# Attention and mixer kernel on one core: the second pair's q is half rotated on VectorE, and the third pair's q is loaded later on SP's queue

## The reference

```python
def rotate(x):
    x1, x2 = (x[..., :half], x[..., half:])
    return np.concatenate([x1 * cos - x2 * sin, x1 * sin + x2 * cos], axis=-1)
q_rot, k_rot = (rotate(q), rotate(k))
scores = scale * np.matmul(q_rot, k_rot.transpose(0, 1, 3, 2))
scores = scores - np.max(scores, axis=-1, keepdims=True)
attn = np.exp(scores)
attn = attn / (np.sum(attn, axis=-1, keepdims=True) + 1e-09)
return np.matmul(attn, v).astype(np.float32)
# mixer
xt = x.transpose(0, 2, 1)
h = np.maximum(xt @ w_tok1, 0.0) @ w_tok2
u = x + h.transpose(0, 2, 1)
h2 = np.maximum(u @ w_ch1, 0.0) @ w_ch2
return (u + h2).astype(np.float32)
```

## Time and profile before

| | us |
|---|---|
| median of three runs | 641.61 |
| the three runs | 641.15, 641.61, 1245.69 |
| profiled execution | 640.87 |
| its span, first to last instruction | 639.1 |
| PE busy / share of the span | 621.5 / 97% |
| DVE busy | 509.4 / 80% |
| ACT busy | 464.2 / 73% |
| POOL busy | 341.0 / 53% |

### The profile page before, as it was taken

How to read it: one execution, slowest core, us unless ns; L and a number is a source line. 1 busy time by engine, 2 the same in 40 slices (tenths; PEclk the granted TensorE clock), 3 DMA queues, 4 the chain that set the end, 5 groups by cost and what they waited for, 6 DMA issues and landing times.

```text
span 639.1 us, 13808 instructions
## 1 busy us (share of the span) xinstructions
PE 621.5 (97%) x4724; PEld 604.7 (95%) x4724; DVE 509.4 (80%) x877; ACT 464.2 (73%) x1016; POOL 341.0 (53%) x316
## 2 busy tenths in 40 slices
PE   3899999999999999999999999999999999999997
PEld 3799999999999999999999999999999999999997
DVE  6899999999999999987385985569935499553895
ACT  3889999988889899986383664776556765567753
POOL 3999999998888887560900002860017800068200
PEclk9999999999999999999999999999999999999999
DMA  4767766767668774406001332000320002100002
GB/s 133 168 159 197 212 151 179 187 173 183 174 176 211 203 189 114 122 20 216 19 1 44 155 84 75 1 2 2 84 74 0 0 0 80 43 33 1 1 3 74
DMA packets 61898, 63.01 MB, mean 99 GB/s; under 512 B 18896, under 2 KB 46160, under 8 KB 61840
## 3 DMA queue, kind: packets, MB, share of 16 engines
q1 hardware_dynamic: 61392, 62.15, 35.7%
q10 hardware_dynamic: 448, 0.10, 0.1%
HBM read 31.46 MB, written 9.44 MB: 64 GB/s over the span
## 4 chain that ended last, share of the span: by engine, by line
PE 95%; SPq 1%; DVE 1%; DMA 1%; ACT 0%; issue 0%; ACTq 0%; DVEq 0%
PE slot L615 12%; PE rest L648 12%; PE rest L625 9%; PE slot L1344 8%; PE slot L1346 8%; PE slot L1345 8%; PE rest L1344 6%; PE rest L1346 6%; PE rest L1345 6%; PE rest L376 3%; PE rest L576 3%; PE rest L635 2%; PE slot L1376 2%; PE rest L1376 2%; PE rest L224 1%; PE rest L221 1%
## 5 line engine op out<-in xcount | busy, mean ns | idle before, releaser
L1335 POOL TENSOR_TENSOR w_ch_part<-w_ch_sums,w_ch_part 128x512 fp32r<-128x512 f32 x21 | 31.0, 1474 | 173.3 <-ACT w_ch_part L1588 173.3
L984 DVE TENSOR_REDUCE neg_max<-slot 128x1 f32<-128x576 f32 x142 | 106.7, 752 | 6.6 <-PE slot L615 2.2
L1652 ACT ACTIVATE pieces<-h 128x288 fp32r<-128x288 f32 x168 | 73.8, 444 | 49.8 <-PE slot L1346 25.3
L992 DVE TENSOR_TENSOR pt_lo<-rest,pt_hi 128x512 fp32r<-128x512 f32 x144 | 96.0, 677 | 1.9 <-ACT pt_hi L845 1.3
L648 PE MATMUL rest<-pt_hi,v 128*128 128x256 f32 (+1 forms) x320 | 89.3, 303 | 0.0
L845 ACT ACTIVATE pt_hi<-rest 128x512 fp32r<-128x512 f32 x144 | 84.1, 595 | 5.2 <-PE rest L625 4.3
L1743 DVE TENSOR_TENSOR pieces<-h,pieces 128x288 fp32r<-128x288 f32 x168 | 74.6, 454 | 9.4 <-ACT pieces L1652 8.9
L648 PE MATMUL rest<-pt_lo,v 128*128 128x256 f32 (+1 forms) x256 | 69.7, 295 | 0.0
L615 PE MATMUL slot<-key,q_hi 128*128 128x288 f32 x252 | 63.5, 333 | 2.2 <-ACT prob_a L838 1.0
L838 ACT ACTIVATE prob_a<-slot,neg_max 128x576 f32<-128x576 f32 x78 | 58.0, 743 | 10.1 <-DVE neg_max L984 10.0
L648 PEld LDWEIGHTS rest<-pt_hi,v 128*128 128x128 f32 x320 | 60.3, 188 | 0.1
(11 more groups left out here) (263 smaller groups left out, 2107.3 us busy)
## 6 DMA issues: line engine op xcount, KB each, us to landing
key<-t_hi_k SPq DMA_DIRECT2D x31, 144.0 KB, 2.3
key<-t_lo_k SPq DMA_DIRECT2D x31, 144.0 KB, 2.4
raw_qk<-in_q_dram SPq DMA_DIRECT2D x16, 256.0 KB, 2.8
raw_v<-in_v_dram SPq DMA_DIRECT2D x16, 256.0 KB, 3.3
x_scratch<-x_pair SPq DMA_DIRECT2D x16, 256.0 KB, 2.1
stage_or_x<-x_scratch SPq DMA_DIRECT2D x16, 256.0 KB, 4.3
q_hi<-t_hi_q SPq DMA_DIRECT2D x31, 128.0 KB, 2.4
q_cross<-t_hi_q SPq DMA_DIRECT2D x31, 128.0 KB, 2.4
```

The costliest lines, as they stand in the source:

```text
L984: dve.tensor_reduce(neg_max[p % 2][:, i:i + 1], slot[g if 2 <= g < 4 else g % 2][:, :, 0:HALF], AX.XY, ALU.max, negate=True).then_inc(maxe ...
L992: dve.tensor_tensor(pt_lo[:, :, cols], rest[:, bank, :].rearrange("p (j n) -> p j n", j=G), f32(pt_hi[:, 0:G, cols]), ALU.subtract).then_i ...
L1652: act.activation(pieces[:, ring(m), 0, :], source[WEIGHTS[n]][:, ft, :], ACT.Copy).then_inc(piece_hi, 1)
```

## The change

`rotate` is cut in two: the products stay in `rotate`, the difference and sum become `rotate_halves`, which `rotate` calls itself except for the second pair's q (m = LENT = 3). There DVE calls it, behind the sixth maximum of the first pair, and POOL waits for `rotated` instead, before it goes on to v. On SP, `load_next("q", 2)` moves from before the loop to behind the second pair's set 0 tiles.

```diff
+    LENT = 3
@@
         eng.tensor_tensor(by_sin[:], x[:], sin, ALU.mult).then_inc(products, 1)
+        if m != LENT:
+            rotate_halves(eng, n, p)
+
+    def rotate_halves(eng, n, p):
+
+        m, half = 2 * p + "kq".index(n), D // 2
         eng.wait_ge(products, m * 2 + 2)
         if p > 0:
             eng.wait_ge(t_ready[n], p)
@@
         load_next("k", 2)
-        load_next("q", 2)
@@
             assemble_q(0, p + 1)
+            if p == 0:
+                load_next("q", 2)
             load_next("k", p + 3)
@@
         rotate(pool, "k", 1)
         rotate(pool, "q", 1)
+        pool.wait_ge(rotated, 2 * LENT + 2)
@@
-        for i in range(1, 7):
+        for i in range(1, 6):
             maximum(0, i)
+        rotate_halves(dve, "q", 1)
+        maximum(0, 6)
         t_part_lo("k", 1, 0)
```

## The result

The change made the kernel slower by 0.8 us: 641.91 us median of 20 runs, against 641.13 of 20 for the kernel before, ratio 1.0013 with a 95% interval of 1.0007 to 1.0019. That is 0.1%, far inside the 2% that the chances speak of, but neither interval includes 1. One of before's 20 runs, at 1245.69 us, is of another kind and enters no ratio. The profiled execution of after took 642.29 us, 640.2 of it span; of before, 640.87 and 639.1.

The account below looks back on a forecast made before the run. The prediction took PE as the chain from 28 us on, its earlier stall coming from SP's issuing. A gain of 0.45 less 0.05 is 0.4 us, from the 641.2 mean to 640.8, range 640.0 to 641.9.

Parts of the forecast that it names:

- the chances: Whole kernel, against a 2% (12.8 us) threshold: 0.01 faster, 0.98 same, 0.01 slower.
- the chain and the head: PE bounds from 28 us on; SP's earlier second-pair tiles shorten PE's early stalls, gaining 0.45 us at the third tile.
- the maximum: DVE's seventh maximum: pushed by the two added instructions from 19.73 to about 20.02, 0.29 us later.
- the high part of q: ACT's instruction for the second pair's q: starts at 21.54 instead of 21.66, only 0.12 us earlier.
- 0.45 less 0.05 is 0.4 us: The forecast's sum: gain at PE's 28.83 wait less the thin-cover allowance, with 0 to 0.6 us as bounds.
- The 0.05 for tiles that land late: Second half of the second pair's tiles: 0.05 us taken off because their cover is only 0.2 us.
- as long as no new wait arises: PE from 28 us on: time won before that point moves the end by the same amount, on this condition.
- The next wait of SP, ahead of the second pair's v and for POOL's split of the first, absorbs the shift on SP.: SP's queue after the second pair's second half: its later issues are made up at this wait.
- the cover of the second pair's second half: Last tile issued at 31.20, landing 33.6 at the median; PE wants it at 33.8, so 0.2 us, the thinnest.
- 640.87 us, 639.1 of it span; so 640.5: Profiled execution of before, less the 0.4 us gain, gives 640.5 us for the changed kernel.
- A: Second pair's second-half tiles land over 2.6 us after issue, PE stalls at 34.27, no gain: 641.1 to 641.3; chance 0.22.
- B: Third pair's late q load holds POOL, PE stalls 1.0 us at its transposes, 0.55 us lost: 641.8; chance 0.10.

Follow-up runs that it names:

- b1: After with third pair's q main load early, its tails behind second pair's tiles, fourth pair's k behind the second half's tiles, mixer weights one pair later: 640.79 us, before 640.97.
- c2: The kernel of b1 run again in another job: 640.98 us median, before 641.05, ratio 0.9999.
- c3: After with only the third pair's q load split: main part early, tails behind the second pair's tiles; 640.90 us, before 641.05.
- a0: The changed kernel run again, with a second profile: 641.77 us median, before 641.03, ratio 1.0011.
- e4: After with the token mixer's weight loads issued one pair later on SP: 640.91 us, before 640.80.
- b2: After with the halves back on POOL, fourth pair's k behind the second half's tiles and mixer weights later; q load late as in after: 641.33 us, before 640.97.
- d2: The kernel of b1 run a third time: 641.08 us median, before 641.09, ratio 0.9999.
- c4: After with fourth pair's k behind the second half's tiles and mixer weights one pair later, q load left late: 641.02 us, before 641.05.
- b3: After with only the fourth pair's k load moved behind the second half of the second pair's tiles: 641.50 us, before 640.97.
- a3: Before with one mixer weight load cut into three transfers, two more SP issues ahead of the fourth pair's tiles: 642.50 us, before 641.03.
- e3: After with 100 already met waits added to PE, so its instruction packets fall elsewhere: 641.89 us, before 640.80.
- the four SP edits: Third pair's q main load early, its tails behind second pair's tiles, fourth pair's k behind the second half's tiles, weights one pair later; in b1 640.79 us.
- c1: The kernel of b1 with the halves of the second pair's q back on POOL: 640.77 us, before 641.05, ratio 0.9993.
- d1: The kernel of c1 run again: 640.69 us median, before 641.09, ratio 0.9994.

## Why the prediction was wrong

**Right: the chain and the head.** PE carries the end: from the second pair's third tile to PE's last instruction it is 606.24 us in before, and 606.18, 606.27 and 606.21 in b1, c2 and c3, which keep all that they win. Each step came out within 0.2 us: DVE's halves at 19.29 (19.10 was read, and POOL was itself 0.24 later in this execution), the maximum at 20.10 (20.02), the high part of q at 21.62 (21.54), the last tile's issue at 23.49 (23.42), PE at 25.92 (25.83) and 28.43 (28.4). In absolute time the third tile is 0.40 us earlier (0.45 was forecast); from PE's first instruction the gain is 0.63 us, and 0.45 in a0. POOL started at 27.58 (27.75), the second half's last tile went out at 30.95 (31.20).

**The step that failed** is the sum, "0.45 less 0.05 is 0.4 us". Its first term held. The 0.05 for tiles that land late measured 0.9 us in the mean span, and a term that was put at nothing, the time around the span, measured 0.34.

**Wrong, first: "as long as no new wait arises" was looked up for 35 us only.** The step was: "The next wait of SP, ahead of the second pair's v and for POOL's split of the first, absorbs the shift on SP." It did: SP goes on with v at 34.25 instead of 34.19, and at 42.49 instead of 42.40. But POOL and SP came out where they were while PE came 0.4 earlier, and the covers behind that point shrink by what PE wins. The working took the cover of the second pair's second half (0.2) and didn't look at the fourth pair's, where SP stands in a row for 14 us. There before's trace gives 1.5 us; PE's gain takes 0.4 of it, and issues that met instruction packets took most of the rest: 0.3 us were left in the one profiled execution and -0.1 in the other.

**Wrong, second: covers were priced with the median landing.** The earlier trace rows showed 4.1 us as the maximum, and the working used it for the rivals alone. A tile with 0.3 us of cover pays 1.2 us when its landing meets a large instruction packet, and where the packets lie isn't seen before the changed kernel has run.

**Wrong, third: the time around the span was kept fixed.** "640.87 us, 639.1 of it span; so 640.5" assumes that the other 1.8 us don't depend on the kernel. They do, by 0.34.

**The rivals.** A and B named two of the three places and a landing beyond the cover as the cause: A's stall is seen in a0 and e4 (34.82 and 35.62), B's in b2 (34.83), not in after. Neither the third place nor the sum of the three was among them.

**The account,** from mean spans less before: with all places covered (b1, c2, d2) -0.48; with q's load late (c4) -0.23; with the fourth pair uncovered too (b3) +0.28; with the second half as well (a0) +0.44. Late landings thus cost 0.92 us together, with an error of 0.2, and with 0.34 outside the span they turn a gain of 0.48 into a loss of 0.78; a0's mean time is 0.76 above before's. How the 0.92 splits is not shown: read one after the other the steps give 0.25 for q's late load, 0.5 for the fourth pair's tile and 0.16 for the second half's, with an error of 0.2 to 0.3 on each. The three places are shown by the stalls themselves (b2; after, a3 and b3; a0 and e4). That packets of instructions make the landings late rests on the table above, in which no landing without one is late, and on e3, where a moved packet made another tile late; no run took the packets away.

The best of these kernels is c1 (d1), with the halves on POOL and the four SP edits: 0.28 and 0.40 us below before. Each interval by itself just includes no difference, so it's likely, not settled. So a gain of the forecast's size came with a better order on SP alone, not with the change.

## What to carry to other kernels

When a bound engine gets earlier, list for the next several rounds what each transfer's issue is anchored on. Those anchored on another engine lose cover by the full gain. Price a cover against the longest landing seen, not the median, and against every place where the issuing queue runs in a row. And compare total times, not only spans: what lies outside may change with the kernel.

## What the runs showed of the hardware

- Packets of instructions run on the DMA engines beside the kernel's transfers: in the first 256 us 16 of 16,384 bytes, of 0.9 to 1.9 us over all traces, and 14 of 8,192 bytes, of 0.3 to 1.4. The last of the five tile transfers landed over 3 us after its issue in 79 of 89 cases with a large packet (median 3.6, up to 4.7), in 2 of 59 with a small one alone, and in none of 443 without.
- In the stalls of after, a3, b3 and e3 one of the 16 parts came 1.3 to 1.7 us behind the other 15.
- At a packet, issues on SP that take 0.6 us elsewhere took 0.8 to 1.9 (before and after, up to 256 us).
- The time outside the span was 1.80 us for kernels with the halves on POOL and 2.14 for those with them on DVE, each within 0.07 of it, in more than 300 runs.
- Two SP issues more in a3, 1.2 us of work some 8 us ahead of a tile with 1.5 us of cover, cost 1.5 us.
